# Order of waits, issues and warm-up matmuls in a linear-attention and two-MLP kernel: GpSimd's waits for VectorE's weight splits dropped, one transfer's queue, two VectorE steps' order and one more warm-up matmul

## The reference

```python
# attention, B=4, H=8, S=768, D=48: a decayed linear recurrence
for t in range(S):
    cur = einsum('bhd,bhe->bhde', u * k[t], v[t])
    y[t] = einsum('bhd,bhde->bhe', r[t], state + cur)
    state = w[:, :, None] * state + einsum('bhd,bhe->bhde', k[t], v[t])
x = y as [3072 tokens, 384 features]
# first MLP: 384 -> 2048 -> 384
h = x @ w_in;  g = max(h, 0) + alpha * min(h, 0);  x = g @ w_out
# second MLP: 384 -> 2048 -> 384
h = x @ w_in2; g = h * tanh(softplus(h));          out = g @ w_out2
```

## Time and profile before

| | us |
|---|---|
| median of three runs | 985.71 |
| lowest and highest | 985.18 and 987.1 |
| the profiled execution | 985.18 |
| its span, first to last instruction | 983.4 |

### The profile page before, as it was taken

One profiled execution on the slowest core, in us unless ns is written; L12 is line 12 of the kernel. 1 busy time (PEld: TensorE's weight loads), 2 busy tenths in 40 slices (PEclk: granted clock), 3 DMA queues, 4 the chain that ended last, 5 costly groups with the idle time before them and its releaser, 6 DMA issues.

```text
span 983.4 us, 24022 instructions
## 1 busy us (share of the span) xinstructions
PE 963.9 (98%) x9504; PEld 784.4 (80%) x9504; DVE 668.6 (68%) x1405; ACT 619.0 (63%) x1274; POOL 372.5 (38%) x664
## 2 busy tenths in 40 slices
PE   7989999999999999999999999999999999999998
PEld 5658778888888888888888888888888888888886
DVE  8897776666666666656653437877777777677775
ACT  6656565445544454555445658878777777787775
POOL 9987687666666676666501430000000000000000
PEclk8999999999999999999999999999999999999999
DMA  6343322112211221111004330100101000000000
GB/s 186 100 142 115 111 62 79 48 52 57 86 46 47 59 80 46 45 46 62 15 8 164 97 125 33 33 3 31 33 33 33 1 32 0 18 14 0 33 1 32
DMA packets 24617, 54.35 MB, mean 55 GB/s; under 512 B 4928, under 2 KB 12736, under 8 KB 24512
## 3 DMA queue, kind: packets, MB, share of 16 engines
q1 hardware_dynamic: 22640, 43.43, 15.1%
q10 hardware_dynamic: 1872, 9.49, 2.4%
HBM read 41.10 MB, written 9.44 MB: 51 GB/s over the span
## 4 chain that ended last, share of the span: by engine, by line
PE 87%; POOL 8%; issue 2%; DMA 1%; SPq 0%; ACT 0%; POOLq 0%; DVE 0%; ACTq 0%
PE acc L1036 39%; PE hid L1020 28%; PE lev L1020 10%; PE lev L1078 6%; POOL arena L305 3%; PE tok L1095 2%; PE tok L1101 2%; POOL arena L455 1%; POOL arena L315 1%; PE tok L1052 1%; POOL arena L482 1%; POOL ruk L468 1%; DMA neg_slope<-slope 1%; POOL ruk L472 1%; POOL w_lo L461 1%
## 5 line engine op out<-in xcount | busy, mean ns | idle before, releaser
L1020 PE MATMUL hid<-x_parts,w_hi 128*128 128x512 f32 x864 | 289.9, 390 | 2.6 <-POOL w_lo L461 1.3
L1036 PE MATMUL acc<-g_hi,w_hi 128*128 128x512 f32 x576 | 230.8, 401 | 0.0
L1036 PE MATMUL acc<-g_hi,w_lo 128*128 128x512 f32 x576 | 224.9, 390 | 0.0
L1020 PEld LDWEIGHTS hid<-x_parts,w_hi 128*128 128x128 f32 x864 | 162.2, 188 | 38.3 <-issue 3.4
L607 DVE COPY_PREDICATED scores<-mask,lev 64x128 f32<-64x128 int8 x420 | 149.8, 357 | 28.9 <-ACT scores L859 17.1
L1020 PE MATMUL hid<-x_parts,w_lo 128*128 128x512 f32 x432 | 168.2, 389 | 0.0
L1036 PE MATMUL acc<-g_lo,w_hi 128*128 128x512 f32 x576 | 162.2, 390 | 0.0
L698 DVE SCALAR_TENSOR_TENSOR hid<-relu_neg,neg_slope,hid 128x512 f32<-128x512 f32 x96 | 72.5, 755 | 124.5 <-ACT hid L905 123.9
L904 ACT ACTIVATE relu_neg<-hid 128x512 f32<-128x512 f32 x96 | 57.2, 596 | 156.6 <-PE hid L1020 154.6
L1036 PEld LDWEIGHTS acc<-g_hi,w_hi 128*128 128x128 f32 x576 | 108.0, 187 | 23.7 <-issue 0.2
L1036 PEld LDWEIGHTS acc<-g_lo,w_hi 128*128 128x128 f32 x576 | 108.1, 188 | 23.0
(11 more groups left out here) (95 smaller groups left out, 1347.0 us busy)
## 6 DMA issues: line engine op xcount, KB each, us to landing
w_raw<-weights SPq DMA_DIRECT2D x32, 384.0 KB, 3.4
arena<-rkv SPq DMA_DIRECT2D x24, 384.0 KB, 3.3
arena<-rk_t SPq DMA_DIRECT2D x48, 192.0 KB, 3.5
arena<-rkv SPq DMA_DIRECT2D x24, 192.0 KB, 2.6
x_dram<-result ACTq DMA_DIRECT2D x6, 768.0 KB, 3.6
arena<-x_dram SPq DMA_DIRECT2D x6, 768.0 KB, 4.4
out<-result ACTq DMA_DIRECT2D x6, 768.0 KB, 3.3
x_parts<-y SPq DMA_DIRECT2D x141, 16.0 KB, 1.8
```

Source lines behind the costliest of these rows:

```text
L1020: last = nc.tensor.matmul(to[:, 0:TILE], w[:, j, kt * P:(kt + 1) * P], x[:, par, kt], start=x is x_hi and w is w_hi and kt == 0, stop=x is ...
L1036: last = nc.tensor.matmul(acc[d][:, 0:TILE], w[:, j, cols], g[:, j % RING], start=j == 0 and g is g_hi and w is w_hi, stop=j == STEPS - 1 ...
```

## The change

Four things are changed; the arithmetic is the same.

1. POOL no longer waits for DVE's splits of slots 5, 7, 9, 11, 13 and 15. It still waits for slot 2 (EARLY - 1) ahead of the queries of chunk 5 and for slot 3 (EARLY) ahead of the keys of its second half.
2. In DVE's first tile, at chunk 4, the state is advanced before the low part of chunk 3's output is made.
3. The small transfer (1, 0) of chunk 3 is issued by SP, in front of its three others, and not by ACT.
4. One more warm-up matmul of 512 columns is executed behind the decay tables.

```diff
-            fill_holes(sp, CHUNKS_PER_TILE - 1, ((0, 0), (0, 1), (0, 2)))
+            fill_holes(sp, CHUNKS_PER_TILE - 1, ((1, 0), (0, 0), (0, 1), (0, 2)))
...
-            def chunk(c, par, uses, last=False, own=(), theirs=((), ())):
-                def step_aside(x):
-                    for i in theirs[x]:
-                        lo_split_reached(pool, i)
+            def chunk(c, par, uses, last=False, slots=()):
                 pool.wait_ge(rows_in[par], 32 * uses)
                 keys_of(c, par, 0)
-                step_aside(0)
+                if isinstance(c, int) and c == CHUNKS_PER_TILE + 1:
+                    lo_split_reached(pool, EARLY - 1)
                 queries_of(c, par, 0)
                 scale_for_state(c, par, uses)
-                for i in own:
+                for i in slots:
                     split_lo(i)
                 rows_for_state(c, par, 0)
                 if isinstance(c, int) and c == CHUNKS_PER_TILE + 1:
                     lo_split_reached(pool, EARLY)
                 keys_of(c, par, 1)
-                step_aside(1)
                 queries_of(c, par, 1)
...
-            chunk(5, 1, 3, theirs=((EARLY - 1,), (EARLY + 2,)))
-            chunk(6, 0, 4, own=(6,), theirs=((7,), (9,)))
-            chunk(7, 1, 4, own=(10,), theirs=((11,), (13,)))
-            chunk(8, 0, 5, own=(14,), theirs=((15,), ()))
+            chunk(5, 1, 3)
+            chunk(6, 0, 4, slots=(6,))
+            chunk(7, 1, 4, slots=(10,))
+            chunk(8, 0, 5, slots=(14,))
...
+                    if x == 0:
+                        advance_state(c, token_bank(0, c))
                     if ends and x == 0:
                         x_lo_part(c - 1, 0, c - 1, token_bank(0, c - 1))
-                    if x == 0:
-                        advance_state(c, token_bank(0, c))
...
-                            fill_holes(act, c - 1, ((1, 0), (1, 1), (1, 2)))
+                            fill_holes(act, c - 1, ((1, 1), (1, 2)))
...
-            for n in (PAIRS, PAIRS // 2):
+            for n in (PAIRS, PAIRS, PAIRS // 2):
                 warm(acc[2], n)
```

## The result

The changed kernel takes 994.61 us in the median (993.52 to 995.62, four runs) against 986.23 for the kernel before: the ratio is 1.0082, 95% interval 1.0064 to 1.0098. Measured a second time it was 1.0067 (1.0047 to 1.0087), 993.31 against 985.91. It is slower by some 7 to 8 us: slower as forecast, by more than the forecast's 4.9, and for another reason than the sum gave. That 994.61 still lies within the range of 982.8 to 995 is luck.

What follows compares the result with a forecast made beforehand. PE was taken as full from 140 to 500 us, so only time ahead of 140 could change. 4.5 (part 1) - 0.2 (parts 2, 3) + 0.6 (part 4) = +4.9: 990.1, median 990.6, range 982.8 to 995.

Steps and rivals of the forecast that it cites:

- the sum: DVE's eight splits between 73.7 and 131 us: 10.4 us more, 5.9 hidden in idle time, 4.5 reaching PE at 131.75.
- Where time can come or go: PE is busy from 140 to 500 us, so time can change only ahead of 140; four waits there, 3.9 us together.
- What part 1 gives: Ahead of 140 us, PE's stalls on POOL's split of slot 10 and DVE's state advance go: at most 2.6 us won.
- the 2.6 us: The most part 1 could win from PE's two 1.3 us stalls; not subtracted, as slot 10's stall was to become DVE's.
- What part 1 costs: DVE's weight splits now run beside POOL's work and grow: 10.4 us more on DVE, 4.5 reaching PE.
- the loss by share: DVE loses 0.59 of each microsecond beside POOL's short instructions, taken as 1.3 us more per split.
- the two meetings: Trace rows at 73.70 and 563.46 where DVE splits began beside a running POOL instruction and took 0.20 and 0.48 us more.
- Starved: DVE is held while POOL's instructions follow one another, from 74.04 on: 10.6 us later, 996 or more; chance 0.10.
- Fair turns: DVE reads at the end of POOL's running instruction; splits' 0.2 to 0.4 us hide: -2.2, 983.5; chance 0.33.
- Parts 2 and 3: At the hand-over, DVE's chain 0.35 us earlier, PE's first `up` 0.2 to 0.6 later: -0.2 taken.
- Part 4: One more warm-up of 512 columns at the start: some 1.7 us long, about 1.1 if the clock rises; +0.6 in the total.
- The total: For the whole kernel, 4.5 - 0.2 + 0.6 = +4.9 us, 990.6 expected of a median.

Runs made afterwards that it cites:

- the kernels with pauses: Part 1 alone (twice) or the whole change, with POOL waiting for its own last result behind each group in chunks 5 to 8: 983.83, 983.40; whole change 983.97 us.
- part 4 alone: The kernel before with only one more warm-up matmul of 512 columns: 985.55 us against 985.65, ratio 0.9991.
- part 1 alone: The kernel before with only POOL's waits for DVE's splits dropped, except slots 2 and 3: 992.02 us against 985.65, ratio 1.0066.
- break_early: As part 1 alone, but POOL waits once for its own queries of chunk 6 (first half): 985.80 us against 985.56, ratio 1.0001.

## Why the prediction came out as it did

- *Where time can come or go.* Right: 140 to 500 us is full in both, and all differences but some 0.3 us lie ahead of 140.
- *What part 1 gives.* Right: the stall on POOL's split of slot 10 went, and that on the advance shrank by 0.9. It was hidden only by the larger loss, and shown by itself in the kernels with pauses (2.6 to 3.6 us less behind the first `up`). The prediction said of the 2.6 us that they "are not taken off"; they are, because the loss sits in one place ahead of them and DVE has caught up by slot 11.
- *What part 1 costs.* This is the step that failed: "the loss by share", 1.3 us for each of eight splits. Of the two ways to read the two meetings the other one was right: DVE stands still until the running POOL instruction ends, less 0.14 us. The step's open question, what happens when POOL's next instruction comes straight behind, has two answers: mostly DVE gets in and POOL waits (42 meetings, as in the rows from 74.91 on), and sometimes it goes on standing still until POOL pauses (six, as in the split of 11.81 us). Slot 7 alone lost 10.9 us, slots 8 and 9 together 1.0, the pair 4, 5 took 0.1 more than before and the pair 12, 13 took 0.2 more than two splits beside an idle POOL, slot 11 nothing. The total on DVE, some 12 us, is near the 10.4 of the sum, but that is luck; one loss of 10.9 cannot hide in many small idle times. Nor did it reach PE where the sum had it, at the `attend` of 131.75, but at an `up` some 30 us earlier that waited for `g_lo`: 5.4 us of stall, and 2.4 for the half clock behind it, a term that the sum did not have. That POOL loses nothing was wrong too (3.88 for 2.44, 1.59 for 1.02).
- *The rivals.* Starved had the mechanism of the loss and the wrong place: it put it at slots 4 and 5, where DVE got in after one instruction. Fair turns had these and most other splits right, and missed the one that made the time.
- *Parts 2 and 3* were put at -0.2 between -0.35 and +0.3. Measured +0.07% with an interval of -0.12% to +0.26%, so neither end is excluded; the trace shows both halves of the argument, the longer wait for the transfer and the vanished one for `g_lo`.
- *Part 4* was put at +0.6. Measured -0.1% with an interval to +0.06%, that is 0.6 at most. That the clock falls all the same was right (to 0.5 from 14 us on in the run of part 4, from 19 on in the changed kernel, where it was 15.5). That the first score comes 1.1 us later held in two profiled executions of the changed kernel (13.07, 13.23, where 11.85 was) and not in the one with part 4 alone.
- *The total.* +4.9 was forecast and +8.4 measured by the medians, +7.4 when the changed kernel was measured once more, and +6.4 for part 1 alone. Behind the first `up` the three profiled executions lie 5.5, 7.2 and 5.9 us above that of before. The 2.5 us ahead of it are well inside what that part varies by itself (63.0 to 71.1 us in the table), so they are put down to no edit; whether parts 2 to 4 add the last 1 to 2 us to part 1's 6.4 the intervals don't tell.

What stays open: what decides whether DVE gets in at the end of a POOL instruction or is passed over; and what causes the breaks in PE's stream. A kernel of only the two instructions, with the length of POOL's run varied, was not tried.

## What to carry to other kernels

Where VectorE and GpSimd both execute instructions with two SBUF inputs, the price is not a share of time: most meetings cost one instruction's rest, and a few cost all that is left of GpSimd's unbroken run, so a single row can carry the whole loss. Look in the timeline for starts that lie before the ends of the row above, and for long runs: the long waits here all met one that was 5.7 us old or more. A wait of GpSimd for its own last result, seen here as 0.08 us of idle time, gave VectorE its turn, and by the medians was some 2 us better than waits for VectorE's work, which hold up all that follows. And when a median moves by less than the first stage varies, compare the time from a later event to the end.

## What the runs showed of the hardware

- A DVE instruction of 0.95 us with two SBUF inputs lasted 11.81, 11.88 and 11.88 us beside a run of POOL instructions with two SBUF inputs, and ended 0.8 us behind the start of the first pause in it, of 0.08 us. The Trainium skill (SBUF — State Buffer, "Who interferes with whom") says that issue order, not op shape, decides who blocks. The rows of slots 4 and 5 agree: the split that began at 74.91 read ahead of POOL's instruction of 75.12. The long split does not: 18 POOL instructions that began behind it, from 86.21 on, went ahead of it. Its one measurement of DVE 6.8 times slower is exceeded here: 12.4 times.
- In 42 meetings, all within 3.2 us of POOL's last idle time, DVE got in at the end of the running POOL instruction though the next came straight behind; the six long ones began 5.7 to 9.0 us after it.
- The granted clock fell to 0.5 during a stall of PE of 5.4 us and stayed there until 104.7; `up` and `attend` behind the stall took 5.58 us for 3.15, so that it cost 2.4 us more than itself.
- Ahead of the first `up`, executions of kernels with the same first 58 us differ by up to 8 us (63.02 to 71.09), by breaks of 1 to 2.2 us in PE's instruction stream with no releaser in the trace, and by falls of the clock behind them (in break_early the mean granted clock was 0.54 from 49.5 to 56.8 us, where the kernel before had the full clock). What causes the breaks is not known.
